# Linear attention and two expert layers on one core: the masked copies of a prologue chunk are moved around the split of the chunk in front

## The reference, cut to what matters

```python
for t in range(S):                                   # q, k, v, alpha: [4, 8, 768, 48]
    state = alpha[:, :, t, :, None] * state + einsum('bhd,bhe->bhde', k[:, :, t], v[:, :, t])
    y[:, :, t] = einsum('bhd,bhde->bhe', q[:, :, t], state)
x = y.transpose(0, 2, 1, 3).reshape(3072, 384)
p = domain_probs / (domain_probs.sum(-1) + 1e-9)
x = sum(p[:, e] * (maximum(x @ w1[e], 0) @ w2[e]) for e in range(4))    # w1: [4, 384, 1024]
h = x @ w_in                                                            # w_in: [384, 2048]
out = (h * clip(h + 3, 0, 6) / 6) @ w_out
```

## Time and profile before

| | |
|---|---|
| median of three runs | 1358.62 us (1358.08 to 1358.93) |
| the profiled execution, its own time | 1358.82 us |
| its span in the trace | 1357.0 us |
| PE busy | 1336.9 us (99%) |
| DVE, ACT, POOL busy | 724.0, 585.1, 781.3 us |
| prologue | 0 to about 64.7 us |

### The profile page before, as it was taken

How to read it: one execution, slowest core, us unless ns; L and a number is a source line. 1 busy time by engine, 2 the same in 40 slices (tenths; PEclk the granted TensorE clock), 3 DMA queues, 4 the chain that set the end, 5 groups by cost and what they waited for, 6 DMA issues and landing times.

```text
span 1357.0 us, 32289 instructions
## 1 busy us (share of the span) xinstructions
PE 1336.9 (99%) x12348; PEld 1091.1 (80%) x12348; DVE 724.0 (53%) x1582; ACT 585.1 (43%) x1238; POOL 781.3 (58%) x862
## 2 busy tenths in 40 slices
PE   7899999999999999999999999999999999999999
PEld 5687788888888888888888888888888888888887
DVE  7857765555555555555555555555555433333333
ACT  5643334333454343355433345433335433335543
POOL 8956766566556655656565655656564344444442
PEclk7999999999999999999999999999999999999999
DMA  5343333333333433333433333343332343333331
GB/s 164 114 146 103 118 118 117 107 117 97 108 118 116 131 105 120 99 110 105 151 105 112 104 109 116 108 137 112 95 98 83 101 125 108 106 93 94 101 121 35
DMA packets 76039, 150.27 MB, mean 111 GB/s; under 512 B 8816, under 2 KB 33648, under 8 KB 75888
## 3 DMA queue, kind: packets, MB, share of 16 engines
q1 hardware_dynamic: 75888, 148.21, 35.9%
HBM read 143.41 MB, written 4.77 MB: 109 GB/s over the span
## 4 chain that ended last, share of the span: by engine, by line
PE 89%; ACT 0%; issue 0%; DVE 0%; ACTq 0%; DVEq 0%
PE psum L672 42%; PE psum L653 40%; PE psum L540 2%; PE psum L532 1%; PE psum L586 1%; PE psum L606 1%; PE psum L576 1%; PE psum L621 1%; PE psum L523 1%; DVE psum L861 0%; DVE x_lo L893 0%; ACT gate L1075 0%; DVE result L897 0%; ACT q_parts L1042 0%; ACT h_hi L1087 0%
## 5 line engine op out<-in xcount | busy, mean ns | idle before, releaser
L1221 POOL TENSOR_TENSOR w_lo<-w_raw,w_hi 128x768 fp32r<-128x768 f32 (+1 forms) x294 | 531.9, 1810 | 531.3 <-ACT w_hi L1094 531.2
L1087 ACT ACTIVATE h_hi<-psum 128x512 fp32r<-128x512 f32 (+1 forms) x288 | 170.9, 594 | 587.7 <-DVE psum L855 506.7
L672 PE MATMUL psum<-h_hi,w_hi 128*128 128x512 f32 x855 | 341.4, 399 | 0.2 <-DVE x_lo L893 0.2
L653 PE MATMUL psum<-x_hi,w_hi 128*128 128x512 f32 (+1 forms) x882 | 339.8, 385 | 0.7 <-issue 0.7
L653 PE MATMUL psum<-x_lo,w_hi 128*128 128x512 f32 (+1 forms) x882 | 339.3, 385 | 0.0
L653 PE MATMUL psum<-x_hi,w_lo 128*128 128x512 f32 (+1 forms) x882 | 339.2, 385 | 0.0
L672 PE MATMUL psum<-h_hi,w_lo 128*128 128x512 f32 x855 | 333.6, 390 | 0.0
L672 PE MATMUL psum<-h_lo,w_hi 128*128 128x512 f32 x855 | 333.0, 389 | 0.0
L855 DVE SCALAR_TENSOR_TENSOR psum<-psum,probs 128x512 f32<-128x512 f32 x184 | 128.5, 699 | 315.1 <-PE psum L653 314.8
L1094 ACT ACTIVATE w_hi<-w_raw 128x768 fp32r<-128x768 f32 x288 | 241.5, 838 | 0.2
L873 DVE TENSOR_TENSOR h_lo<-psum,h_hi 128x512 fp32r<-128x512 f32 x280 | 192.9, 689 | 46.5 <-ACT h_hi L1087 46.3
(11 more groups left out here) (81 smaller groups left out, 964.0 us busy)
## 6 DMA issues: line engine op xcount, KB each, us to landing
w_raw<-w SPq DMA_DIRECT2D x288, 384.0 KB, 3.1
alpha_q<-qa SPq DMA_DIRECT2D x48, 256.0 KB, 3.9
k_raw<-kk SPq DMA_DIRECT2D x48, 128.0 KB, 3.5
probs<-prob_scratch SPq DMA_DIRECT2D x24, 256.0 KB, 3.7
v_sb<-v SPq DMA_DIRECT2D x48, 96.0 KB, 2.8
out<-result SPq DMA_DIRECT2D x18, 256.0 KB, 3.8
level_sb<-level SPq DMA_DIRECT2D x1, 128.0 KB, 3.1
ident_sb<-ident SPq DMA_DIRECT2D x1, 64.0 KB, 2.9
```

Source lines behind the costliest of these rows:

```text
L653: mm = pe.matmul(h_bank[g % 2][:, cols], a, x[:, cols], start=k == 0 and i == 0, stop=k == K3 - 1 and i == 2)
L672: mm = pe.matmul(out_bank[k], a, x, start=first and i == 0, stop=(last or g == PLAIN - 1) and i == 2, skip_group_check=ph == 0)
L1087: act.activation(h_at(h_hi, x_hi, g)[:, cols], h_bank[g % 2][:, cols], ACT.Relu if g < PLAIN else ACT.Copy).then_inc(hh_made, 1)
L1221: op = pool.tensor_tensor(w_lo[:, g % RING, cols], w_raw[:, g % RAW, cols], w_hi[:, g % RING, cols].bitcast(F32), ALU.subtract)
```

## The change

The change rewrites DVE's list in the prologue. Nothing is added or taken away; the lists of PE and SP are the same, and ACT's and POOL's instructions stand in the same order as before. Before, the body of the loop for chunk `n` began with chunk `n`'s four masked copies, three query steps woven between them (for the last chunk `keep(7, 0)` stood ahead of the split of chunk 6 already). Now chunk 0's four masked copies stand ahead of the loop; for every chunk behind it `keep(n + 1, 0)` stands ahead of `split_x(n)`, and `keep(n + 1, 1..3)` behind it and behind query step 5. Query steps 0 to 2 follow one another without masked copies between them, and query step 6 comes after `keep(n + 1, 3)`.

```diff
             for step in range(3, Q_STEPS):
                 scale_q(1, step)
+            for step in range(keeps(0)):
+                keep(0, step)
             for n in range(PER_TILE):
                 last = n >= PER_TILE - 2
                 ahead = PER_TILE if last else n + 2
                 at = 4 * (n - PER_TILE + 2) if last else 0
                 beside, behind = ((2, 2), (2, 0))[n - PER_TILE + 2] if last else (3, 2)
-                if n == PER_TILE - 1:
-                    for step in range(1, keeps(n)):
-                        keep(n, step)
-                    for step in range(beside):
-                        scale_q(ahead, at + step)
-                else:
-                    for step in range(keeps(n)):
-                        keep(n, step)
-                        if step < beside:
-                            scale_q(ahead, at + step)
+                for step in range(beside):
+                    scale_q(ahead, at + step)
                 at += beside
                 for g in early_after(n - 1):
                     hidden_lo(g, early=True)
                 for step in range(behind):
                     scale_q(ahead, at + step)
                 if n < PER_TILE - 1:
                     next_state(n)
                 turn_y(n)
+                if n < PER_TILE - 1:
+                    keep(n + 1, 0)
+                split_x(n)
                 if not last:
                     scale_q(ahead, at + behind)
-                if n == PER_TILE - 2:
-                    keep(n + 1, 0)
-                split_x(n)
                 if n == PER_TILE - 1:
                     next_state(n)
+                else:
+                    for step in range(1, keeps(n + 1)):
+                        keep(n + 1, step)
                 if not last:
                     scale_q(ahead, at + behind + 1)
```

## The result

The changed kernel takes 1362.22 us (median of 15 runs, 1360.64 to 1363.19), the kernel before 1359.06 (15 runs beside them, 1358.08 to 1362.39). The ratio is 1.0015, with a 95% interval of 1.0008 to 1.0022. It is slower: the medians differ by 3.2 us, the ratio says 2, its interval 1 to 3; I had predicted +0.5 and a range that ends at 1361.0.

The account below looks back on a forecast made before the run. POOL was taken to set the prologue's pace, PE to bound the rest. Minus 0.28 plus 0.5 (caught) or 1.2 (missed) gave +0.2 or +0.9; taking +0.5 on 1358.62 gave 1359.1 us, range 1357.4 to 1361.0.

Parts of the forecast that it names:

- the 1.62 us: PE's idle time ahead of chunk 3's output: would close there but open ahead of chunk 5's scores, gaining nothing.
- POOL's wait ahead of `decays(4, 1)`: Early prologue, waiting for chunk 2's query step 6: idle 0.5 to 1.4 us instead of 0.29, delay arriving whole at chunk 7.
- the missed case: Step 5 of chunk 2 misses the gap between `w_lo` halves and waits for the second's end: POOL 1.2 us late.
- the border: Instant between POOL's two `w_lo` halves, about 20.4 us, uncertain by about 0.1; step 5's margin there is 0.06.
- In a chunk at POOL's pace there is room for both.: Later prologue chunks: copies ahead of query steps 5 and 6 fit, about 1.8 us needed after an output, about 3.5 available.
- as many query steps as before meet as many POOL instructions: Prologue: argument against POOL going faster, whose pace differs by 0.54 us from chunk to chunk.
- The gain of 0.28: Chunk 7's scores could start at 53.94 instead of 54.22, 0.14 behind the end of `k_top`: 0.28 us gained.
- The path from POOL to the end: From POOL through chunk 7's `k_top` and scores to the first full hidden tile: delay arrives whole, last stretch 10.47 us.
- The clock: Rival, chance 0.07: PE's clock falls in a gathered wait of some 2.2 us, +4 us, or rises late, 1 to 2.
- POOL is not held up: Rival, chance 0.27: POOL merely on time in the prologue gives -0.3 us, or goes faster for a gain of 1.0.
- the masked copies do bound it: Rival, chance 0.08: the 1.62 us ahead of chunk 3's output and its like in chunks 4 and 5 come through, -2 to -4.
- All three signs by which I would be wrong: Prologue: scores well after `k_top`'s end, other POOL waits for DVE, or a stretch behind chunk 7's scores not 10.5 us.

Follow-up runs that it names:

- the first kernel of experiment 4: Changed kernel with additional warm-up calls and four more behind chunk 4's key transpose: 1361.48 us, ratio 1.0010 to the kernel before.
- experiment 4: Changed order plus additional warm-up: four further calls, `w_lo` in four pieces, or changed order for chunks 0 and 1 alone; ratios 1.0010, 1.0006, 1.0000 to the kernel before.
- the filled kernel before: Kernel before with eight warm-up calls instead of four, and two instead of one behind key transposes of chunks 1 to 4: 1358.83 us, ratio 0.9991; repeated 1360.89, 1.0002.
- experiment 3: Additional warm-up calls on kernel before, changed kernel, changed with three decay buffers, kernel before with three: 1358.83, 1362.43, 1361.02, 1360.38 us, beside 1360.83 for the kernel before.
- the bunched order: Kernel before with each chunk's four masked copies side by side ahead of query steps 0 to 2: 1362.88 us, ratio 1.0021 to the kernel before.
- the woven order: Kernel before with masked copies of chunks 1 to 6 one place earlier, a query step still between each two: 1358.92 us, ratio 0.9993 to the kernel before.
- experiment 1: Parts of the change against the kernel before: step 6 directly behind step 5, 1.0029; changed order for chunks 0 and 1 alone, 1.0015; all but chunk 1, 1.0012.
- the four pieces: Changed order with additional warm-up calls, POOL making `w_lo` in four pieces instead of two: 1361.02 us, ratio 1.0006 to the kernel before.
- three buffers: Three decay buffers instead of two: changed kernel 1362.06 us (1.0011); with additional warm-up, changed kernel 1361.02 (1.0005), kernel before 1360.38 (1.0000).
- experiment 5: Masked copies side by side, or one place earlier with query steps between, on the kernel before: 1.0021 and 0.9993; with additional warm-up 1.0025 and 0.9997.

## Why the prediction was wrong

**Right:** nothing of the 1.62 us reached the end. POOL's wait ahead of `decays(4, 1)` is the first loss; I gave 0.3 or 1.2 us late, it was 1.01, the missed case: step 5 of chunk 2 stood from 20.79 us beside the second half of `w_lo`, which ended at 21.23. (The 0.1 us by which I called the border uncertain I took from no row; half of the pair's 2.13 us instead of 1.0 moves it by 0.07.) The main part is unchanged. In the profiled execution the shift of the first full tile is the shift of the span.

**The step that failed** is the sentence "In a chunk at POOL's pace there is room for both." I had priced the bare copies (3 x 0.32) and what stands ahead of step 5, found room on the path from an output to the next scores, and did not add up DVE's whole chunk. It had 0.81 us of idle time in 6.91. The new order asks for 1.08 more, so DVE becomes the bound, from chunk 3 on, at 7.2 us. Half of the 1.08 I could have read: 0.39 for copies without cover, and 0.17 for query step 2 (0.22 before, 0.39 after), which waits for steps 0 and 1 as a copy waits for the last. The other half comes of who meets POOL's long instructions: steps 0 and 1, with slack, met `w_lo` before; now step 6 does, which POOL waits for, and steps 3 and 4, ahead of the state. I took the meetings as a coin toss at one border and as equal in number afterwards ("as many query steps as before meet as many POOL instructions").

How the loss builds up is read from where DVE takes the state of each chunk. In the profiled executions of the change the clock is mixed in. A pair with the clock up from 20.3 and 20.5 us on is the first kernel of experiment 4 against the filled kernel before of experiment 3, one execution of each. At chunk 3:

```profile
39.95 0.34 DVE L835 TENSOR_TENSOR state<-state_decayed,psum 128x192 f32<-128x192 f32 x1
```

```profile
37.87 0.35 DVE L835 TENSOR_TENSOR state<-state_decayed,psum 128x192 f32<-128x192 f32 x1 [0.37 <-PE psum L621]
```

| us later, at the state of chunk | 1 | 2 | 3 | 4 | 5 | 6 | first full tile |
|---|---|---|---|---|---|---|---|
| changed kernel, profiled execution | 2.27 | 3.05 | 3.40 | 3.32 | 4.03 | 3.72 | 3.44 |
| pair with the clock up | 0.08 | 0.92 | 2.08 | 2.37 | 2.71 | 2.82 | 2.86 |

In the profiled execution 3.05 of the 3.44 us are there by chunk 2, from POOL's first wait and the late clock together. With the clock up, 0.92 are there by chunk 2, and the other 1.94 come where DVE is the bound. So the step above accounts for most of the loss where the clock plays no part, and for a small part of this one profile. The spans of the pair differ by 2.2 us (1359.6 and 1357.4): here 0.7 us were made up behind the first full tile.

That putting the copies side by side is enough for the loss is shown by the bunched order, which moves nothing around a split and loses 1.0021. That moving copies a place forward costs nothing as long as they keep their cover is shown by the woven order, 0.9993. The change's own place, all of them ahead of query step 6, was not run with cover; that it is not needed for the loss is also seen in experiment 1. How the 1.08 us divide between bare waits and meetings with `w_lo` is read from the rows and was not varied alone; the four pieces changed both engines at once.

**The gain of 0.28** at chunk 7's scores was not there: they started 1.33 us behind the end of `k_top`, not 0.14, and that `k_top` came 3.02 late.

**The path from POOL to the end** was too simple as well. I let a delay of POOL arrive whole. With the changed order for chunks 0 and 1 alone and the clock up (experiment 4), POOL waited 1.64 us once, and the scores of chunk 7 were 0.98 late against the filled kernel before (54.95 against 53.97), but the first full tile only 0.24 (64.70 against 64.46): the rest was made up behind the scores, in a stretch that I had held at 10.47 us.

**The clock** was in the rivals at 0.07. Its late rise, to 29 us, belongs to the profiled execution, and with it POOL's second wait: where the clock was up (the first kernel of experiment 4), POOL waited 1.63 us ahead of `decays(4, 1)` and not at all ahead of `decays(5, 1)`. In its four runs with a mean clock of 1.000 the changed kernel took 1360.64 to 1363.19, where the kernel before, in the five sets, took 1358.38 to 1361.14 with that clock; so the loss does not need it. It did fall once in a gathered wait of PE, the one of 3.62 us.

**The rivals:** "POOL is not held up" fell with the first row; "the masked copies do bound it" fell too. The true case, DVE as the new bound, was not among them. All three signs by which I would be wrong came: scores well after `k_top`'s end, more waits of POOL, and a last stretch of 9.98 us instead of 10.5.

What stays open: whether three buffers cost the old order anything, and why runs of one kernel with the same mean clock differ by up to 5 us (the kernel before beside experiment 5, with 0.999: 1358.17 and 1363.25). PE's idle time in and ahead of an output, which the profile puts to issue (0.64 us before at 57.4, 1.47 with three buffers, 1.35 ahead of chunk 3's output in the changed kernel, 1.62 in the bunched one), varies between executions, but I did not vary it; it may be a part of that spread.

## What to carry to other kernels

Before moving instructions on an engine that is not the bound, add up its whole cycle from start to start, with the idle time in it, and re-price each instruction for its new neighbours: in these rows, a masked copy costs DVE 0.20 us behind a query step and 0.33 behind the copy that it waits for. Where instructions of one engine are stretched beside a long one of another, what counts is which of them meets it: let it be one that nobody waits for. And read the clock, and repeat both kernels in one set, before believing a difference of 1 to 2 us.

## What the runs showed of the hardware

Several DVE instructions with both inputs in SBUF took far longer beside POOL's subtraction of 384 columns (1.0 us) whatever their own size: an addition of 24 columns 0.98 us, a query step of 128 columns 1.04, where both take 0.2 to 0.3 alone. The masked copies, which read PSUM and a mask, were not: in the changed kernel's prologue those of levels 1 to 3 took 0.29 to 0.45 us, those of the diagonal 0.71 to 0.74.

TensorE's clock in the first 30 us differs between executions. The profiled one of the kernel before ran at 1.2 GHz from 8.6 to 22.2 us and has a mean clock of 0.995; others of the same kernel have 1.000. The filled kernel before was at 1.2 GHz from 13.6 to 20.5 us in one execution (1359.25 us) and from 12.3 to 22.5 and again from 39.6 to 43.0 in another (1360.89 us). In its second set two groups of runs lie 2.4 us apart and go with the mean clock; in its first set they do not go with it strictly (1358.83 us with 0.995, 1360.12 with 0.997).
